# u of batches 3 to 6 by seven block products of half sums, and v's tiles normalised on ScalarE

## What is computed

```python
kv = einsum('bhsd,bhse->bhde', k, v); o = einsum('bhsd,bhde->bhse', q, kv)
x = o / sqrt(mean(o * o, -1) + 1e-6) * g_norm            # heads joined: 8 x 576 x 512
h = maximum(x @ w_in, 0); u, v = h[..., :512], h[..., 512:]
v_n = (v - mean(v)) / sqrt(var(v) + 1e-6)                # over the 512 features of a row
x = (u * (w_spatial @ v_n + b_spatial)) @ w_out
h = maximum(x @ w_in2, 0)
y = (h * sigmoid(conv3(h))) @ w_out2                     # conv3: three taps along the sequence
```

## Time and profile before

| | |
|---|---|
| median of three runs | 790.61 us (790.01 to 791.25) |
| the profiled execution's own time | 789.98 us |
| its span | 788.0 us |
| TensorE busy | 779.9 us, 99% |
| VectorE busy | 583.4 us, 74% |
| ScalarE busy | 421.8 us, 54% |
| granted TensorE clock, mean | 0.999 |
| chain that ended last | TensorE 91%, VectorE 3%, DMA 3%, ScalarE 1% |

### The profile page before, as it was taken

The page is one execution under the profiler, slowest core; times in us unless marked ns, Lnnn a source line. Parts: engine busy times, 40 slices in busy tenths (PEclk is TensorE's granted clock), DMA queues, the critical chain, the costliest instruction groups (busy, mean ns, idle before and its releaser), DMA issues.

```text
span 788.0 us, 15294 instructions
## 1 busy us (share of the span) xinstructions
PE 779.9 (99%) x5654; PEld 702.0 (89%) x5654; DVE 583.4 (74%) x1262; ACT 421.8 (54%) x753; POOL 29.4 (4%) x40
## 2 busy tenths in 40 slices
PE   9999999999999999999999999999999999999997
PEld 7679789798998979899999898998989899898986
DVE  3765785867577474757899989497985979689791
ACT  4664362644335253442457767375774757567562
POOL 4342000000000000000000000000000000000000
PEclk9999999999999999999999999999999999999999
DMA  9872629556252642213092212221021212102102
GB/s 325 306 254 67 245 92 296 208 193 233 76 209 86 195 150 61 106 46 99 23 364 74 106 42 105 68 104 56 7 109 58 105 53 101 57 14 105 54 0 67
DMA packets 35005, 96.92 MB, mean 123 GB/s; under 512 B 2738, under 2 KB 9106, under 8 KB 30228
## 3 DMA queue, kind: packets, MB, share of 16 engines
q1 hardware_dynamic: 33476, 90.09, 33.7%
q10 hardware_dynamic: 1488, 6.30, 2.1%
HBM read 66.11 MB, written 30.28 MB: 122 GB/s over the span
## 4 chain that ended last, share of the span: by engine, by line
PE 91%; DVE 3%; DMA 3%; ACT 1%; issue 1%; SPq 1%; ACTq 0%; DVEq 0%
PE ps L642 25%; PE ps L457 25%; PE ps L634 21%; PE ps L483 11%; PE ps L426 2%; PE ps L410 2%; PE ps L490 2%; PE ps L561 1%; DMA work<-w_out_T_dram 1%; DMA sq_then_r<-r_scratch 1%; PE ps L436 1%; DVE vrr L1115 0%; DVE h_and_sums L1285 0%; DVE t_then_s L1185 0%; PE ps L549 0%
## 5 line engine op out<-in xcount | busy, mean ns | idle before, releaser
L642 PE MATMUL ps<-w_in_split,v_hg_split 128*128 128x512 f32 x832 | 194.9, 390 | 0.0
L642 PEld LDWEIGHTS ps<-w_in_split,v_hg_split 128*128 128x128 f32 x832 | 155.7, 188 | 32.2
L457 PE MATMUL ps<-w_sp_split,v_hg_split 128*128 128x288 f32 x896 | 120.1, 295 | 0.0
L457 PEld LDWEIGHTS ps<-w_sp_split,v_hg_split 128*128 128x128 f32 x896 | 119.3, 188 | 0.0
L457 PE MATMUL ps<-x_operand_split,w_in_split 128*128 128x288 f32 x768 | 103.8, 296 | 0.0
L457 PEld LDWEIGHTS ps<-x_operand_split,w_in_split 128*128 128x128 f32 x768 | 102.1, 188 | 0.7 <-issue 0.2
L483 PE MATMUL ps<-w_in_split,x_operand_split 128*128 128x512 f32 x384 | 92.1, 393 | 1.6 <-DVE work L1136 1.6
L483 PEld LDWEIGHTS ps<-w_in_split,x_operand_split 128*128 128x128 f32 x384 | 71.1, 188 | 19.1 <-issue 3.1
L1285 DVE TENSOR_TENSOR h_and_sums<-h_and_sums,ps 128x288 f32<-128x288 f32 x160 | 68.4, 449 | 7.7 <-PE ps L634 7.2
L1136 DVE TENSOR_TENSOR work<-ps,work 128x576 f32<-128x576 f32 x32 | 24.0, 756 | 66.6 <-PE ps L457 66.5
L1285 DVE TENSOR_TENSOR h_and_sums<-work,ps 128x288 f32<-128x288 f32 x64 | 28.2, 450 | 46.8 <-PE ps L634 46.3
(11 more groups left out here) (124 smaller groups left out, 1066.8 us busy)
## 6 DMA issues: line engine op xcount, KB each, us to landing
kv_raw<-kv_main_dram SPq DMA_DIRECT2D x8, 2048.0 KB, 11.8
q_raw<-q_T_dram SPq DMA_DIRECT2D x8, 1152.0 KB, 5.1
operand_scratch<-t_then_s SPq DMA_DIRECT2D x8, 1152.0 KB, 4.7
operand_raw<-operand_scratch SPq DMA_DIRECT2D x8, 1152.0 KB, 5.5
sq_then_r<-r_scratch SPq DMA_DIRECT2D x14, 576.0 KB, 7.0
operand_scratch<-work SPq DMA_DIRECT2D x24, 288.0 KB, 2.7
operand_more_raw<-operand_scratch SPq DMA_DIRECT2D x8, 864.0 KB, 7.2
w_out_split_scratch<-v_hg_split ACTq DMA_DIRECT2D x2, 2048.0 KB, 13.9
```

Of the source, the lines that this page charges most:

```text
L457: last = pe.matmul(pair[bank][:, c, :], st, mo[:, c * HALF:(c + 1) * HALF], start=(n == 0), stop=(n == len(steps) - 1))
L642: last = pe.matmul(PS[:, ROW_BANK[i], :], x, wout2[:, w, F_ORDER[e], :], start=(e == 0 and n == 0), stop=(e == FT - 1 and n == len(PASSES) ...
```

## The change

In batches 3 to 6 u is made by the seven products too: weights and x of the batch are taken as 2 x 2 blocks, each product is six matmuls of 288 columns, and there are two groups of feature rows, so 84 matmuls in place of 96. ScalarE copies the first product of a group out, VectorE adds up seven sums per group (`u_sums`) into u without a relu, and the relu goes into the gate (`fast_gate`, one operation with a maximum and a product). T1 to T4 of a batch are differences of x's blocks: made raw after x's low parts in the batch before (`u_t_raw`), split on ScalarE (`u_t_hi`) and VectorE (`u_t_lo`). The raw T's lie where w_out2 was, so those of batch 3 wait for its store. S1 to S4 of w_in are combined at the start (`u_combine_weights`) and split in batch 1. Batches 0, 1, 2 and 7 keep the four-tile form.

In every batch the normalised tile of v is now made by ScalarE (`v_scale`: v times 1/std plus minus mean times 1/std) ahead of its high part; VectorE only makes that second column. SyncE's loop is written out, and the load of K and V (`load_kv`) waits until sq_then_r has landed.

```diff
+FAST = 3
+FAST_BANK = [6, 7, 1, 0, 2, 3, 4, 5]
+FAST_GATE = [2, 3, 0, 1]
...
-            with sp.Fori(0, B - 3) as b:
+            for b in range(B - 3):
                 sp.wait_ge(s_o, (b + 2) * MT)
                 load_q(b + 2)
                 spread_r(b + 1)
+                sp.wait_ge(s_rB, (b + 1) * CH * DMA)
                 sp.wait_ge(s_kv, b + 3)
                 load_kv(b + 3)
                 store_gated(b)
...
+            def fast_product(b, g, k, ahead, two_ahead):
+                n = g * NPROD + k
+                if n == 2:
+                    pe.wait_ge(s_vr, b * NT + 2)
+                elif n == 3:
+                    pe.wait_ge(s_vr, b * NT + 4)
+                elif n == 4:
+                    pe.wait_ge(s_vr, (b + 1) * NT)
+                elif n == 6 and ahead:
+                    pe.wait_ge(s_ms, b + 2)
+                elif n == 7 and two_ahead:
+                    pe.wait_ge(s_kvd0, b + 3)
+                    pe.wait_ge(s_kvd1, b + 3)
+                elif n == 8:
+                    pe.wait_ge(s_ux1, b * U_GROUPS - FAST * U_GROUPS + 1)
+                elif n > 8:
+                    pe.wait_ge(s_usum, fast_u(b) + LAST_SUM[n - 8])
+                a, t = PRODUCTS[k]
+                if g == 0 and t in U_T_ORDER:
+                    pe.wait_ge(s_UTlo, fast_t(b) + U_T_ORDER.index(t) + 1)
...
+            def v_scale(b, p):
+                v = v_sb[p % 2] if V_TILES[p] < FULL else v_sb[p % 2][0:REST, :]
+                n = P if V_TILES[p] < FULL else REST
+                act.wait_ge(s_nmr, b * NT + p + 1)
+                act.activation(v, v, ACT.Identity, bias=nmr[0:n, :], scale=vrs[0:n, :]).then_inc(s_vn, 1)
...
-                dve.tensor_scalar(v_sb[p % 2][0:n, :], v_sb[p % 2][0:n, :], mv[0:n, 0:1], vrs[0:n, :],
-                                  ALU.subtract, ALU.mult).then_inc(s_vn, 1)
+                dve.tensor_scalar(nmr[0:n, :], vrs[0:n, :], mv[0:n, 0:1], -1.0, ALU.mult, ALU.mult).then_inc(s_nmr, 1)
...
+            def u_t_raw(a):
...
+                if isinstance(a, int) and a == FAST:
+                    dve.wait_ge(s_wo2_st, 2 * DMA)
...
+            def fast_gate(b, m):
+                if m == 0:
+                    dve.wait_ge(s_usum, fast_u(b) + U_PRODUCTS)
+                dve.wait_ge(s_sp, b * MT + m + 1)
+                dve.scalar_tensor_tensor(out=whole(u_sb[m]), in0=whole(u_sb[m]), scalar=0.0, in1=pair[FAST_GATE[m]],
+                                         op0=ALU.max, op1=ALU.mult).then_inc(s_g, 1)
...
+            def fast_body(b, two_ahead, make_t):
+                for i in range(NT):
+                    v_stats(b, i)
+                    if i == NT - 1:
+                        mean_square(b + 1)
+                    if i:
+                        v_lo(b, i - 1)
+                    v_normalise(b, i)
+                    if i == 0:
+                        u_t_lo(b, T3)
+                u_t_lo(b, T4)
+                if two_ahead:
+                    kv_copy(b + 2)
+                inverse_root(b + 1)
+                v_lo(b, NT - 1)
+                u_sums(b, 0)
+                u_sums(b, 1)
+                for m in range(MT):
+                    x_scale(b + 1, m)
+                fast_gate(b, 0)
+                for m in range(MT):
+                    x_lo(b + 1, m)
+                fast_gate(b, 1)
+                if make_t:
+                    u_t_raw(b + 1)
+                fast_gate(b, 2)
+                if make_t:
+                    u_t_lo(b + 1, T2)
+                    u_t_lo(b + 1, T1)
+                fast_gate(b, 3)
+                t_a(b)
+                t_b(b)
+                t_c(b)
```

More of the change, by code:

```diff
@@ L532, in body @@
                     pe.wait_ge(s_winu, MT)
-                for m in range(MT):
-                    if m == 3 and two_ahead:
-                        pe.wait_ge(s_kvd0, b + 3)
-                        pe.wait_ge(s_kvd1, b + 3)
-                    u_product(b, m, ahead)
+                if fast:
+                    for g in range(U_GROUPS):
+                        for k in range(NPROD):
+                            fast_product(b, g, k, ahead, two_ahead)
+                else:
+                    for m in range(MT):
+                        if m == 3 and two_ahead:
+                            pe.wait_ge(s_kvd0, b + 3)
+                            pe.wait_ge(s_kvd1, b + 3)
+                        u_product(b, m, ahead)
                 if first:
@@ L774, in body @@
                     kv_copy(b + 2)
+                if fast:
+                    u_t_hi(b, T4)
+                    u_first_copy(b, 0)
+                    v_hi(b, NT - 1)
+                    u_first_copy(b, 1)
+                    for m in range(MT):
+                        x_hi(b + 1, m, True)
+                    if make_t:
+                        for t in U_T_ORDER[:3]:
+                            u_t_hi(b + 1, t)
+                    return
                 u_relu(b, 0)
@@ L791, in body @@
                         x_hi(b + 1, m)
+                    if isinstance(b, int) and b == 1:
+                        for n in range(4):
+                            u_weight_hi(n)
+                    if make_t:
+                        for t in U_T_ORDER[:3]:
+                            u_t_hi(b + 1, t)
                 else:
@@ L903, in _ @@
             kv_copy(1)
[L904 to L909 removed]
+            body(0, True, True, False, False)
+            body(1, True, True, False, False)
+            body(2, True, True, False, True)
+            with act.Fori(FAST, B - 2) as b:
+                body(b, True, True, True, True)
+            body(B - 2, True, False, True, False)
             def operand_hi(b, k):
@@ L1131, in v_lo, with u_combine_weights @@
                     dve.tensor_tensor(vnA[REST:P, :], v[0:REST, :], vnA[0:REST, :].bitcast(F32), ALU.subtract).then_inc(s_vlo, 1)
+            def u_combine_weights(n):
+                a11, a21 = wu_raw[:, 0:2, 0:HALF_D], wu_raw[:, 0:2, HALF_D:F1]
+                a12, a22 = wu_raw[:, 2:4, 0:HALF_D], wu_raw[:, 2:4, HALF_D:F1]
+                raw = u_weight_unsplit
+                if n == 0:
+                    dve.wait_ge(s_winu_in, DMA)
+                    dve.tensor_tensor(raw[S1], a21, a22, ALU.add).then_inc(s_US, 1)
+                    dve.tensor_tensor(raw[S3], a11, a21, ALU.subtract).then_inc(s_US, 1)
+                    dve.wait_ge(s_US, 1)
+                    dve.tensor_tensor(raw[S2], raw[S1], a11, ALU.subtract).then_inc(s_US, 1)
+                else:
+                    dve.wait_ge(s_US, 3)
+                    dve.tensor_tensor(raw[S4], a12, raw[S2], ALU.subtract).then_inc(s_US, 1)
@@ new lines, in u_t_lo, with u_add, u_sums, own @@
+            def u_t_lo(a, t):
+                dve.wait_ge(s_UThi, fast_t(a) + U_T_ORDER.index(t) + 1)
+                dve.tensor_tensor(u_operand[t][LO], u_t_unsplit[t], u_operand[t][HI].bitcast(F32), ALU.subtract).then_inc(s_UTlo, 1)
+            def u_add(b, g, dst, x, k, product):
+                dve.wait_ge(s_up, fast_u(b) + g * NPROD + product + 1)
+                dve.tensor_tensor(dst, x, PS[:, FAST_BANK[(g * NPROD + k) % 8], 0:HALF], ALU.add).then_inc(s_usum, 1)
+            def u_sums(b, g):
+                def own(n):
+                    dve.wait_ge(s_usum, fast_u(b) + g * NPROD + n)
+                top, low = u_sb[g], u_sb[2 + g]
+                dve.wait_ge(s_ux1, b * U_GROUPS - FAST * U_GROUPS + g + 1)
+                if g:
+                    own(0)
+                else:
+                    for s in s_go:
+                        dve.wait_ge(s, DMA * b)
+                    dve.wait_ge(s_T, b * 4)
+                u_add(b, g, a_u2, a_x1, 1, 1)
+                u_add(b, g, top[:, 0:HALF], a_x1, 2, 2)
+                own(1)
+                u_add(b, g, a_u4, a_u2, 3, 3)
+                u_add(b, g, a_u3, a_u2, 5, 5)
+                own(3)
+                u_add(b, g, top[:, HALF:S], a_u4, 4, 5)
+                own(4)
+                u_add(b, g, low[:, HALF:S], a_u3, 3, 5)
+                u_add(b, g, low[:, 0:HALF], a_u3, 6, 6)
@@ L1167, in body @@
                         x_lo(b + 1, m)
+                    if isinstance(b, int) and b == 1:
+                        for n in range(4):
+                            u_weight_lo(n)
+                    if make_t:
+                        u_t_raw(b + 1)
                 else:
```

161 lines of the change are left out of this document (124 added, 37 removed).

## The result

| | before | changed |
|---|---|---|
| median of the runs on one chip | 790.50 us (790.01 to 791.25, four runs) | 800.62 us (799.40 to 801.74, four runs) |
| ratio | | 1.0126, 95% interval 1.0110 to 1.0142 |
| span of the profiled execution | 788.0 us | 797.6 us |
| TensorE, VectorE, ScalarE busy | 779.9, 583.4, 421.8 us | 778.4, 620.9, 455.8 us |

What follows compares the result with a forecast made beforehand. It took TensorE to bound the kernel, with VectorE's hand-overs becoming late after the change. Batches 3 to 5 (6.3), batch 6 (1.9) and batch 2 (0.7) summed to 8.9 us: 799.0 us forecast, range 792.5 to 804.5.

Steps and rivals of the forecast that it cites:

- VectorE's load, +9.1 us: VectorE's busy time per batch rises from 30.1 to 39.2 us, net of removed normalises and added sums and T blocks.
- r at 27.2: In a fast batch VectorE finishes r 27.2 us after v's first tile starts, where it was 25.25; ends 26.0 to 28.2.
- The scale's terms, 1.1 + 0.6 - 0.4: Delay of r: tile 1's low part 1.1 later, 64-row tile's low part waits 0.6, last normalise gives back 0.4.
- The first statistics: Start of VectorE's work on v; a 1 us push by gate 3 and the t block counted only in r's high end.
- The sums: First sum starts at 27.8 to 28.2; product 9 waits 2.0 us, product 11 0.3 more; spatial products end at 47.5.
- Round trip and gate 2: r to DRAM and back takes 10.7 us, landing at 37.9; 11.1 us of VectorE work then ends gate 2 at 49.0.
- Gate 2 ends at 49.0 ... and starts the next batch at 49.0: TensorE, done at 47.5, waits for this gate: +2.2, taken as +2.1 in each of batches 3 to 5, 6.3 us.
- Batch 6: Without a kv product, product 6 waits 2.4 for T4's low part, products 9 and 11 0.9 and 0.2: +1.9 us.
- Batch 2: Raw differences for batch 3 wait for the w_out2 store ahead of gate 2: 0 to 2.0 us, taken as 0.7.
- At nothing: Parts priced at zero: combining w_in, low weights in batch 1, SyncE's written-out loop, and batch 7, where only the normalise moves.
- The last step of the sum: 8.9 on the profiled 789.98 gives 798.9; the runs' median is 0.6 above that execution; forecast stated as 799.0 us.
- the full saving: Rival: gate 2 ends by 45.2 and the first sum comes by 26.2, so nothing is late; 784.2 us, chance 0.10.

Runs made afterwards that it cites:

- The last version: Changed kernel with VectorE normalising, K and V copy on ScalarE, two T low parts moved, batch 6 plain, gate 2 before raw differences: 785.55 us, ratio 0.9947.

## Why the prediction was right, and where it was not

- **Sign and size** came from its mechanism: VectorE's work late for TensorE at the first sum and at the end of the batch, worth more than 1.6 us of products. VectorE's load, +9.1 us, was met (39.2 forecast, 39.10).
- **r at 27.2** was 27.6, and that is near by luck: two errors offset each other. From the first statistics to r it is 22.75 us for 21.47 before, 1.3 longer and not 2.0. All of it is the scale's: with the scale alone it is 22.69, and with the normalise back on VectorE 21.47, T4's low part included, for which the prediction had added 0.7 (no run has it with the first statistics on time, so how much of it the late start hides stays open). The scale's terms, 1.1 + 0.6 - 0.4, were right in sum, although one scale takes 0.80 to 0.82 us and not 0.69: two columns as scale and bias cost more than the row with one had suggested. The Trainium skill's page ScalarE: Activation LUTs (section "What ACT_TABLE_LOAD costs") gives 186 ns plus 0.833 ns per element and 93 for each column, an estimate of 799 ns for 512 elements; the trace agrees, 804 ns the median of 40. The other 0.9 us are the next point. Another 0.16 is the starting point: the prediction counted from 229.67, TensorE's timeline has that batch start at 229.51.
- **The first statistics**: the prediction took them as hardly delayed and kept as the high end of r that gate 3 and the t block push them. They did, to 4.86 us after the batch's start from 3.94 (233.45 less 229.51). This is the link that closes the ring.
- **The sums**: first sum at 28.2 for 27.8. Product 9 waited 1.56, not 2.0, because it was due at 27.2 instead of 26.2 after short gaps at T4, at the K and V copy and at the start. The spatial products ended near 48.1, not 47.5.
- **Round trip and gate 2**: 10.1 for 10.7, the lower bound of the range, and 10.8 us from x_scale to gate 2's end for 11.1. Gate 2 ended at 48.5 for 49.0, and the wait at v's first tile was 0.5 to 0.8 instead of about 1.5; x_scale waited 3.7 to 4.0 for the 4.5 named. Batches 3 to 5: +5.8 for +6.3.
- **The step that failed in its reason** is "Gate 2 ends at 49.0 ... and starts the next batch at 49.0". It made gate 2's place the cause of the period. The edit that moved it left the period as it was; the path goes on past gate 2 through the t block into the next batch. By gate 2 alone the period would be about 47.6, an estimate from the rows: 3.94 to the first statistics, 22.75 to r, 10.08 of trip and 10.82 to gate 2's end. So +2.1 a batch for the +1.8 to +2.1 measured is in part luck: the 0.7 for T4 and the 0.6 too much of trip stood in for the 0.9 of the late statistics.
- **Batch 6**: +2.3 for +1.9, from T4's low part (2.61 late for 2.4) and the sum (0.51 for 0.9), with 0.8 of short gaps where 0.2 was forecast. **Batch 2**: +0.2 for +0.7; the store landed in time because the load came behind the trip, which the run without that order shows.
- **At nothing** was wrong twice. Batch 7 and what follows lost 1.6, and the scale alone brings 1.5 of it: a longer chain was counted as free because only an operation was moved. The weight combining cost nothing that shows: it takes 2.9 us where VectorE had waited 2.51 (L1266 to L1269), and v's first tile starts at 40.86 for 40.36, but in the kernel before with only SyncE's loop changed it starts at 40.86 too. SyncE's loop gained 1.2 in batch 0 of the kernel before; with both, batch 1 starts 0.4 early. So +1.6 and -0.4 here, and -0.5, +0.4 and -0.5 at the three terms above, lead from 8.9 to 9.6 (rounding included).
- **The last step of the sum** is off by 0.5: the median of the kernel before is 790.61, and with 8.9 on it that is 799.5, not the 799.0 that was said. Measured 800.62.
- Of the rivals, the full saving needed both hand-overs 2 to 4 us sooner. The last version does that, with five edits; its batches are 1.3 us shorter each.

## What to carry to other kernels

When work is added to an engine that is not the bound, add up the whole ring that the engine closes from one iteration to the same point of the next, round trips included, and compare it with the bound engine's period; a busy share of 80% says nothing of it. If the ring is the longer one, moving a wait within it only changes where the wait shows, and only less serial work or a shorter trip helps; once the path runs through the other engine's wait, the same reordering pays. The chain that ended last tells which of the two it is: look whether it passes through the bound engine within a batch. An operation that changes engines has to be costed in every iteration whose cover differs, the last one above all.
